# Suffix products instead of reciprocals in a linear attention with two dense layers, r made on VectorE, and a new order of the beginning

## The reference

```python
# r, k, v, w: (4, 8, 768, 48) float32, w in 0.8..0.95; u: (8, 48)
state = zeros(4, 8, 48, 48)
for t in range(768):
    cur = outer(u * k[t], v[t])
    y[t] = r[t] @ (state + cur)
    state = w[t][:, None] * state + outer(k[t], v[t])
x = y as (3072, 384)
h = x @ w_in                       # (384, 2048)
x = (h * clip(h + 3, 0, 6) / 6) @ w_out
xn = x / sqrt(mean(x * x) + 1e-6) * rms_g
out = (silu(xn @ w_gate) * (xn @ w_val)) @ w_out2   # 384 -> 1536 -> 384
```

## Time and profile before

| | |
|---|---|
| median of 3 runs | 933.13 us (932.55 to 935.83) |
| the profiled execution | 935.66 us, its span 933.9 us |
| TensorE matmuls busy | 921.6 us, 99% of the span |
| VectorE, ScalarE, GpSimd busy | 521.3, 361.7, 291.9 us |
| mean granted clock of TensorE | 0.998 of full |
| DMA | 60.4 MB, 65 GB/s over the span |

### The profile page before, as it was taken

How to read it: one execution, slowest core, us unless ns; L and a number is a source line. 1 busy time by engine, 2 the same in 40 slices (tenths; PEclk the granted TensorE clock), 3 DMA queues, 4 the chain that set the end, 5 groups by cost and what they waited for, 6 DMA issues and landing times.

```text
span 933.9 us, 17547 instructions
## 1 busy us (share of the span) xinstructions
PE 921.6 (99%) x7064; PEld 772.9 (83%) x7064; DVE 521.3 (56%) x752; ACT 361.7 (39%) x786; POOL 291.9 (31%) x244
## 2 busy tenths in 40 slices
PE   7999999999999999999999999999999999999998
PEld 7899988888888888888888888888888888888886
DVE  6888976566666666315774553553463373363332
ACT  4557454354444445336463123223223223223212
POOL 4789544454454444324351011011011001101000
PEclk9999999999999999999999999999999999999999
DMA  9874442233223231014221010010000001000000
GB/s 255 237 208 129 109 131 60 63 105 86 75 61 107 69 83 51 22 39 135 86 83 45 0 35 34 1 34 34 0 34 35 1 19 50 0 1 34 1 1 34
DMA packets 33008, 60.40 MB, mean 65 GB/s; under 512 B 6112, under 2 KB 19936, under 8 KB 32928
## 3 DMA queue, kind: packets, MB, share of 16 engines
q1 hardware_dynamic: 27104, 50.82, 18.7%
q10 hardware_dynamic: 5824, 8.47, 3.1%
HBM read 47.66 MB, written 9.44 MB: 61 GB/s over the span
## 4 chain that ended last, share of the span: by engine, by line
PE 93%; DVE 4%; issue 1%; DMA 1%; ACT 1%; SPq 1%; DVEq 0%; ACTq 0%
PE acc L1079 34%; PE bank L1050 11%; PE bank L1052 11%; PE bank L1051 11%; PE pair L1050 5%; PE pair L1051 5%; PE pair L1052 5%; DVE ki L731 1%; PE acc L1113 1%; PE pair L1132 1%; PE pair L1189 1%; PE pair L1161 1%; DVE cum L719 1%; PE bank L1068 1%; PE bank L1153 1%
## 5 line engine op out<-in xcount | busy, mean ns | idle before, releaser
L1079 PE MATMUL acc<-gs,w_dn 128*128 128x512 f32 (+1 forms) x1512 | 357.0, 382 | 1.2 <-issue 1.2
L1079 PEld LDWEIGHTS acc<-gs,w_dn 128*128 128x128 f32 x1512 | 272.9, 188 | 55.1 <-issue 1.3
L945 POOL TENSOR_TENSOR gs<-act_g,gs 128x512 fp32r<-128x512 f32 (+1 forms) x96 | 122.1, 1272 | 208.3 <-ACT gs L550 208.2
L1050 PE MATMUL bank<-xs,w_up 128*128 128x512 f32 (+1 forms) x459 | 171.9, 374 | 1.4 <-DVE state L762 1.2
L1052 PE MATMUL bank<-xs,w_up 128*128 128x512 f32 (+1 forms) x459 | 169.1, 368 | 0.0
L1051 PE MATMUL bank<-xs,w_up 128*128 128x512 f32 (+1 forms) x459 | 169.0, 368 | 0.0
L801 DVE SCALAR_TENSOR_TENSOR act_g<-act_u,bank 128x512 f32<-128x512 f32 (+1 forms) x112 | 67.5, 603 | 139.8 <-ACT act_u L542 139.8
L869 DVE TENSOR_TENSOR act_u<-act_u,bank 128x512 f32<-128x512 f32 x72 | 49.5, 688 | 146.8 <-ACT act_u L612 146.8
L542 ACT ACTIVATE act_u<-bank,half 128x512 f32<-128x512 f32 (+1 forms) x112 | 70.0, 625 | 150.8 <-PE bank L1052 139.9
L616 ACT ACTIVATE gs<-act_g 128x512 fp32r<-128x512 f32 x72 | 45.5, 632 | 155.9 <-DVE act_g L875 155.9
L1050 PEld LDWEIGHTS bank<-xs,w_up 128*128 128x128 f32 x459 | 86.4, 188 | 18.0 <-DVE state L762 1.6
(11 more groups left out here) (121 smaller groups left out, 1121.6 us busy)
## 6 DMA issues: line engine op xcount, KB each, us to landing
rkn<-in_rkN SPq DMA_DIRECT2D x22, 384.0 KB, 4.1
rkt<-in_rkT SPq DMA_DIRECT2D x44, 192.0 KB, 3.6
val<-in_valN SPq DMA_DIRECT2D x22, 256.0 KB, 3.0
x<-x_dram SPq DMA_DIRECT2D x6, 768.0 KB, 4.2
dec<-in_decT SPq DMA_DIRECT2D x46, 97.5 KB, 2.3
x_dram<-xo SPq DMA_DIRECT2D x5, 768.0 KB, 4.1
out<-xo SPq DMA_DIRECT2D x5, 768.0 KB, 3.3
raw_dn<-in_w_out SPq DMA_DIRECT2D x14, 192.0 KB, 4.8
```

The lines of the kernel that those rows point to most:

```text
L945: pool.tensor_tensor(gs[:, f % GRING, 1, tok], act_g[:, f % 2, tok], gs[:, f % GRING, 0, tok].bitcast(F32), ALU.subtract).then_inc(s_glo, 1)
L1050: pe.matmul(dst, w_hi, x_hi, start=first, stop=False)
L1079: last = pe.matmul(ps_o[m][:, tok], w[:, wp, m * P:(m + 1) * P], gs[:, f % GRING, xp, tok], start=f == 0 and a == 0, stop=f == nf - 1 and ...
```

## The change

For each group VectorE now scans the decay backwards (`prep_suffix`), which gives for each token the product of the decays after it (`after`) and for the whole chunk (`whole`). k is multiplied by the first. One small reciprocal of `whole` (8 columns) starts a second, forward scan (`prep_prefix`) whose result, cum / whole, is written over `dec` and multiplied with r. So four reciprocals of 128 columns leave, one scan comes in. r is made by VectorE (`prep_r` there, in phase PREP behind `prep_k`) for groups 2 and later; GpSimd makes it for groups 0 and 1. The state is scaled by the `whole` of the group that comes next, for all groups.

The order of the beginning changes. TensorE: the 30 unused products become 3 wide and 7 narrow ones; `sums(0)` goes behind the first hidden product, `keys(1)` into step 2. ScalarE: `place_val3`, the copy of the keys of group 0 and half of the fills of group 1 go to VectorE, the keys of group 1 to step 2. VectorE: `update_state(0)` and `scale_state(0)` go into steps 0 and 2. Loads: ScalarE issues w_in 0 to 2 and u and no more; SP issues the decay of group 2, waits for both masks (`s_mask` 2), and issues all else behind them. The decay is always loaded with 64 rows in the half 0 (130 KB instead of 97.5), and the decay of group g + 4, no longer g + 5, is loaded in INV1(g).

```diff
@@ sync
-                need(sp, s_cum, g - 1)
+                need(sp, s_rd, g - 1)
...
                 if phase == INV1:
-                    if g + 5 < GROUPS:
-                        load_dec(g + 5)
                     if g + 4 < GROUPS:
+                        load_dec(g + 4)
                         load_rk(g + 4)
...
             sp.dma_start(rms_s[:, :], rms_g).then_inc(ldG, 16)
-            landed(sp, ldR, 1, 2)
-            for b in range(PB):
-                sp.dma_start(u_b[T * b:T * (b + 1), :], u[b].partition_broadcast(T)).then_inc(ldU, 16)
+            load_dec(2)
+            sp.wait_ge(s_mask, 2)
             load_rkn(2)
-            load_dec(2)
+            load_up(sp, EARLY_UP)
+            load_dn(sp, 0)
             load_rk(2)
-            sp.wait_ge(s_ki, 2)
-            for f in range(FIRST_UP, FIRST_UP + 2):
+            load_dn(sp, 1)
+            for f in range(EARLY_UP + 1, FIRST_UP + 2):
                 load_up(sp, f)
                 load_dn(sp, f - 2)
             load_dec(3)
...
@@ scalar
-            for f in range(FIRST_UP):
+            for f in range(EARLY_UP):
                 load_up(act, f)
-                if f < 2:
-                    load_dn(act, f)
+            for b in range(PB):
+                act.dma_start(u_b[T * b:T * (b + 1), :], u[b].partition_broadcast(T)).then_inc(ldU, 16)
...
-            for g in range(2):
-                copy_bonus(g)
-                for part in range(2):
-                    fill_bonus(g, part)
-                place_val3(g)
-                if g == 0:
-                    copy_keys(0)
-            for g in range(2):
-                keep_last(g)
-            for f in range(2):
-                split_up(f)
+            copy_bonus(0)
+            for part in range(2):
+                fill_bonus(0, part)
+            copy_bonus(1)
+            fill_bonus(1, 0)
+            split_up(0)
             x1_hi(0, 0)
-            split_up(2)
+            split_up(1)
             x1_hi(1, 0)
-            copy_keys(1)
-            for f in range(3, FIRST_UP):
+            for f in range(2, FIRST_UP):
                 split_up(f)
...
@@ vector
+                backwards = (t.rearrange("p a b t -> p (a b t)")[:, ::-1] for t in (
+                    dec[0:DP, q, :, :, :], first1[0:DP, :, :, :]))
+                dve.tensor_tensor_scan(suffix[0:DP, q, 0:CHUNKS][:, ::-1], *backwards, 1.0,
+                                       ALU.mult, ALU.add).then_inc(s_suf, 1)
...
+            def prep_prefix(g):
+                q = slot(g)
+                dve.wait_ge(s_suf, g + 1)
+                need(dve, s_cum, g)
+                dve.reciprocal(whole1[0:DP, :, :, 0:1].rearrange("p a b t -> p (a b) t"), whole(g)).then_inc(s_inv, 1)
+                dve.wait_ge(s_inv, g + 1)
                 dve.tensor_tensor_scan(*(t.rearrange("p a b t -> p (a b t)") for t in (
-                    cum[0:DP, q, :, :, :], dec[0:DP, q, :, :, :], first1[0:DP, :, :, :])), 1.0,
+                    dec[0:DP, q, :, :, :], dec[0:DP, q, :, :, :], whole1[0:DP, :, :, :])), 1.0,
                                        ALU.mult, ALU.add).then_inc(s_cum, 1)
-                for p in ((0,), (1, 2, 3))[part]:
-                    dve.reciprocal(ki[0:DP, q, p, :, :], cum[0:DP, q, p, :, 1:T1]).then_inc(s_inv, 1)
...
+            def prep_r(g):
+                q = slot(g)
+                dve.wait_ge(s_cum, g + 1)
+                dve.wait_ge(p_y, g - 1)
+                dve.tensor_tensor(rd[0:DP, q, :, :, :].rearrange("p a b t -> p (a b) t"),
+                                  rkt[0:DP, q, 0, :, :, :].rearrange("p a b t -> p (a b) t"),
+                                  dec[0:DP, q, :, :, 0:T].rearrange("p a b t -> p (a b) t"), ALU.mult).then_inc(s_rd, 1)
...
                         prep_k(g + 2)
+                        prep_r(g + 2)
                 if phase == INV1 and g + 3 < GROUPS:
-                    prep_scan(g + 3)
-                if phase in (INV1, INV2) and g + 3 < GROUPS:
-                    prep_inv(g + 3, phase - INV1)
+                    prep_suffix(g + 3)
+                if phase == INV2 and g + 3 < GROUPS:
+                    prep_prefix(g + 3)
...
             for g in range(2):
-                mask_scores(g)
+                place_val3(g)
+            copy_first_keys()
+            mask_scores(0)
+            fill_half()
+            mask_scores(1)
             for g in range(2):
                 x1_lo(g, 0)
-            update_state(0)
             for f in range(NF1):
                 hidden(0, f)
                 if f == 0:
-                    prep_scan(2)
-                if f < 2:
-                    prep_inv(2, f)
+                    update_state(0)
+                    prep_suffix(2)
+                if f == 1:
+                    prep_prefix(2)
                 if f == 2:
+                    scale_state(0)
                     sum_bonus(2)
                     prep_k(2)
+                    prep_r(2)
...
@@ tensor
             pe.wait_ge(s_ones, 1)
-            busy(20)
+            busy(3, 4)
+            busy(5, 1)
             bonuses(0)
-            busy(3)
             pe.wait_ge(const, NCONST)
             scores(0)
             keys(0)
-            busy(3)
+            busy(2, 1)
             bonuses(1)
-            pe.wait_ge(s_bonus, 1)
-            sums(0)
-            busy(4)
             scores(1)
             outputs(0)
             outputs(1)
-            pe.wait_ge(s_bonus, PLACED)
-            keys(1)
```

More of the change, by code:

```diff
@@ L212, in columns, with after, whole @@
             return slice(g % B * C, (g % B + 1) * C)
-        def is_first(g):
-            return g < SETS
+        def after(g):
+            return suffix[0:DP, slot(g), 2:2 + CHUNKS].rearrange("p (c t) -> p c t", t=T1)[:, :, 0:T]
+        def whole(g):
+            return suffix[0:DP, slot(g), 0:CHUNKS].rearrange("p (c t) -> p c t", t=T1)[:, :, 1:2]
         def has_state(g):
@@ L513, in keep_last @@
             def keep_last(g):
-                act.wait_ge(s_cum, g + 1)
-                act.activation(last[0:DP, g % LASTS, :], cum[0:DP, slot(g), :, :, T:T1].rearrange("p a b t -> p (a b t)"),
-                               ACT.Copy).then_inc(s_last, 1)
+                act.wait_ge(s_suf, g + 1)
+                act.activation(last[0:DP, g % LASTS, :].unsqueeze(2), whole(g), ACT.Copy).then_inc(s_last, 1)
             def copy_keys(g):
@@ L736, in prep_k @@
                 landed(dve, ldR, g, 2)
-                dve.wait_ge(s_inv, PAIRS * (g + 1))
-                dve.tensor_tensor(*(t.rearrange("p a b t -> p (a b t)") for t in (
-                    ki[0:DP, q, :, :, :], rkt[0:DP, q, 1, :, :, :], ki[0:DP, q, :, :, :])), ALU.mult).then_inc(s_ki, 1)
+                dve.wait_ge(s_suf, g + 1)
+                need(dve, p_sc, g - 1)
+                keys_taken(dve, p_kt, g - 2)
+                dve.tensor_tensor(ki[0:DP, q, :, :, :].rearrange("p a b t -> p (a b) t"),
+                                  rkt[0:DP, q, 1, :, :, :].rearrange("p a b t -> p (a b) t"), after(g), ALU.mult).then_inc(s_ki, 1)
+            def prep_r(g):
[5 more added lines that the diff above has]
+                                  dec[0:DP, q, :, :, 0:T].rearrange("p a b t -> p (a b) t"), ALU.mult).then_inc(s_rd, 1)
             def mask_scores(g):
@@ L846, in attention @@
                 if phase == PREP:
-                    if has_state(g) and not is_first(g):
+                    if has_state(g):
                         scale_state(g)
@@ L884, in _ @@
             dve.memset(first1[:, :, :, 0:1], 1.0).then_inc(s_first1, 1)
+            dve.memset(suffix[:, :, CHUNKS:CHUNKS + 2], 1.0).then_inc(s_const, 1)
+            dve.memset(whole1[:, :, :, 1:T1], 0.0).then_inc(s_const, 1)
             dve.wait_ge(s_first1, 2)
             dve.tensor_scalar(ones[:, :].rearrange("p (b t) -> p b t", b=PB), first1[:, 0, :, 1:T1], 0.0, 1.0, ALU.mult, ALU.add).then_inc(s_ones, 1)
+            dve.wait_ge(s_const, 2)
             for g in range(2):
-                prep_scan(g)
-                for part in range(2):
-                    prep_inv(g, part)
+                prep_suffix(g)
+                prep_prefix(g)
                 prep_k(g)
@@ L966, in prep_r @@
                 pool.wait_ge(s_cum, g + 1)
-                need(pool, p_y, g - 1)
                 pool.tensor_tensor(*(t.rearrange("p a b t -> p (a b) t") for t in (
-                    rd[0:DP, q, :, :, :], rkt[0:DP, q, 0, :, :, :], cum[0:DP, q, :, :, 0:T])), ALU.mult).then_inc(s_rd, 1)
+                    rd[0:DP, q, :, :, :], rkt[0:DP, q, 0, :, :, :], dec[0:DP, q, :, :, 0:T])), ALU.mult).then_inc(s_rd, 1)
             def attention(phase, g):
@@ L1235, in run1 @@
                             keys(g + 1)
+                    if (e, f) == (0, 0):
+                        pe.wait_ge(s_bonus, PLACED)
+                        sums(0)
                     if (e, f) == (0, 2):
-                        sums_read(pe, 0)
+                        keys(1)
```

85 lines of the change are left out of this document (41 added, 44 removed).

## The result

The changed kernel takes 941.09 us (median of 6 runs, 939.46 to 941.54 without one disturbed run) against 933.3 us (median of 6) of the kernel before. The ratio is 1.007, 95% interval 1.0054 to 1.0085: slower by 5 to 8 us. The two medians differ by 7.8 us, but 85 later runs of the kernel before have medians of 934.5 to 934.7 us, so that the 6.5 us of the ratio is the better size. I had forecast 933.8 us and a range of 928.8 to 937.5; both the time and the likeliest case (no change that can be measured) were wrong.

The account below looks back on a forecast made before the run. TensorE, busy 921.6 of 933.9 us, was taken to bound the kernel. Terms of +2.0 (transfers), +0.5 (half clock), -1.2 (state waits) and -0.6 (instruction wait) gave +0.7 on 933.13: 933.8 us, range 928.8 to 937.5.

Parts of the forecast that it names:

- the likeliest case: Whole kernel: no measurable change, an effect below about 0.5% (4.7 us); chance 0.72, against faster 0.15 and slower 0.13.
- Masks: Beginning, VectorE in line with GpSimd: second mask ends at some 18.0 us against 17.7 before, bounds 17.0 and 20.2.
- First hidden product: Beginning, TensorE: starts at about 19.5 us instead of 22.66, if its wait for instructions is gone.
- the instruction wait: Beginning, TensorE stopped from 17.71 to 20.46 us, read as waiting for instructions behind data: 2.75 us, expected gone.
- Transfers: Loads behind SP's wait: piece 6 of w_in lands at 32.5 us, 5.5 later; step 5 starts +2.0 us, bounds -4.5 and +4.2.
- Clock: Half clock after TensorE idles 3 to 4 us ahead of group 1's sums: +0.5 us, bounds 0 and +1.7.
- The 0.5 us that I had for piece 7: Steps before step 5: piece 7 of w_in lands 2.3 us behind piece 6, delaying step 5 by 0.5 us more.
- 60 to 120 us: TensorE's waits there: VectorE's state waits go, -1.2 us (0 to -1.8); half an instruction wait goes, -0.6 (-1.2 to +1.2).
- 120 us on: Steady part to 560 us: VectorE's saving of 1.4 us per group is worth nothing, since TensorE is full.
- Sum: Whole kernel: +2.0 + 0.5 - 1.2 - 0.6 = +0.7 us on the median 933.13, giving 933.8 us.
- Rival B: SP's wait opens late, since VectorE loses to GpSimd and masks end at 20.2 us: +5.9, 939.0 us; chance 0.08.
- Rival A: Early start is kept, by transfers in time or masks by 17.0 us: 927.4 us, partly lost 930; chance 0.18.

Follow-up runs that it names:

- e12: The kernel before with only its unused TensorE products cut, from 30 of 128 columns to 3 of 512 and 7 of 128; 932.52 us, ratio 0.9974.
- e1: The changed kernel with SP waiting for its loads for r and k of group 1 instead of for both masks; 934.48 us, ratio 1.0009.
- e3: The kernel before with one line added: SP waits for both masks ahead of its loads for group 2; 936.53 us, ratio 1.0018.
- e11: The changed kernel, its wait for both masks kept, with 28 unused TensorE products of 256 columns instead of 3 of 512 and 7 of 128; 940.10 us.

## Why the prediction was wrong, point by point

**Masks.** Forecast 18.0 us, measured 18.15. Working through the line of VectorE and GpSimd was right within 0.6 us at every row. By the Trainium skill (SBUF — State Buffer, SBUF: two separate sides) such instructions lock each other out; the trace agrees, with 2.30 us for a scan of 1.23. I had missed one place: two copies of 96 columns, one input each, took 1.29 us beside GpSimd's r, where I had 0.5.

**First hidden product.** Forecast 19.5, measured 20.57 us; the instruction wait went as forecast. The outputs ran at 1.2 GHz, which I had not forecast.

**Transfers: the first of two terms that failed in size.** This is the term for piece 6 (32.5 us) in the +2.0 us. The place and the chain were right: piece 6, ScalarE's split, the fills, the 3.6 us gap ahead of the sums of group 1. I had +2.0 us for the start of step 5, without the clock; measured +4.5 with it. Piece 6 landed at 34.0 us instead of 32.5. The rate was no cause: the engines moved 271 GB/s from 18.2 to 34.0 us, where I had 262. That is 4.28 MB, and only 3.38 MB stood ahead of piece 6. I took the queue as served in order of issue. The landings are in that order (the next transfer, issued at 26.64 us, landed at 34.5), but by these bytes 0.9 MB of the transfers issued behind piece 6 must have been moved before it was whole: +3.3 us at this rate, worked out and not seen packet by packet. The mean of 271 GB/s holds the idle start already, so my 1.6 us for that and 0.4 us for the rate come off, which leaves 1.3 of the 1.5 us.

**Clock: the second.** I had +0.5 us, for six products. The half clock lasted from 35.5 to 42.2 us and covered three blocks: the sums of group 1 took 1.03 us instead of 0.61, the products of w_out behind them 2.37 instead of 1.64, and step 5's own products put its activation 1.0 us further back (5.5 us late, the first product 4.5). So the half clock behind the 3.6 us gap cost some 2.2 us, four times what I took and above my bound of 1.7. From the start of the fills to step 5 it took 4.2 us before and 5.74 here (34.45 to 40.19); 0.4 us of the difference are not the clock but the copy of the keys of group 1 in ScalarE's queue, a term that I had left out though the change puts it there. The 0.5 us that I had for piece 7 was not paid. This closes the step: 2.5 forecast, + 1.5 for the transfers, + 1.7 for the clock, + 0.4 for the copy, - 0.5, is 5.6, and 5.5 was measured.

**60 to 120 us.** Forecast -1.2 for the state and -0.6 for the instruction wait, measured -1.0 for both together. The wait for the state did not go (1.0 us in two waits), the instruction wait of 1.2 us did. e12 makes the same stretch from step 5 to pass 2 in 81.5 us with the old arithmetic, the changed kernel in 82.5, e1 in 81.8, before in 83.5. So the cheaper VectorE work, for which I had -1.2 us, gave nothing there that can be shown; the 1.2 us instruction wait explains what was gained. That this one went is luck in my sum, where it stood at half its size.

**120 us on.** No effect, as forecast, up to the last output copy: there the two traces are 4.5 us apart, and 4.4 at pass 2.

**Sum.** In the span: +5.5 at step 5, -1.0 to pass 2, and 0.8 at the very end. This last is in every version with the new arithmetic: the span ends 2.8 to 3.1 us after SP's last issue in these eleven, and 2.2 us in before, e3 and e12. In the same eleven, and not in the three, a packet of another instruction queue (q14) runs beside the last output. That it is the cause is not shown, but the 0.8 us go with the program's instructions and not with the beginning, and no term of mine had them. The two medians of six differ by 7.8 us and not by 5.3, since before's profiled execution was 2.4 us above its median. Rival B had 939.0 us, but its mechanism, late masks, did not occur. Rival A did not occur either; in e1, without the wait, the early start is kept, and the median is only that of before.

**Rivals of the explanation.** That the clock of the beginning was the cause is refuted by e11, where it stays up and the loss stays too, and by e1, where the loss goes with the clock still down for 6.7 us. That the wait for the masks protects the instruction fetch is refuted by e1 for the changed kernel; in the kernel before it does so (e3). Why is e1 3.6 us ahead of before at pass 2, and its median no better? Its profiled execution was its fastest (932.73 us, 1.75 below its median), before's lay 1.0 above that of the set, and 0.8 us are lost at the end: together 3.6 us. What the slower executions of e1 lose, and where, was not seen.

## What to carry to other kernels

A wait put ahead of prefetches is paid by the consumer with the least spare time (piece 6 had 0.5 us, and in the changed kernel the last 3.8 us of waiting cost 5.2), the more so where an in-order queue processes the prefetch ahead of urgent work; price the clock behind the new gap as well. When a change bundles a saving on engines that don't bound with a new order of the beginning, judge the two apart: the saving of 31 us on VectorE was worth nothing that could be shown, and taking one line out of the new order gave back all of the loss. The same line in the kernel before stretched the same steps by as much and cost only 2 us, since it also let TensorE's instructions through: read what a line does from the stretch in which it acts. In a beginning full of DMA, count TensorE's instructions too.

## What was not expected of the hardware

- TensorE's granted clock fell to 0.50 at 11.5 us, behind 3.5 us in which matmuls were busy 2.16 us, and stayed there until 25.1 us, while TensorE was 94% busy by the profile. By the Trainium skill (TensorE: Matmul & The Clock Gate, Part 1) half rate is the state after idling and full rate comes back with sustained work; here 12.67 busy us in 13.50 did not bring it back, where in e1 it came back at 19.6 us, behind 6.47 busy us in 6.70.
- Of the kernel before and e12 the one with the longer half clock (6.8 us against 3.4) is the faster: 932.52 against 934.48 us.
- A 192 KB transfer took 8.6 us from issue to landing with 271 GB/s moving, 2.8 us more than the same piece before.
- TensorE stood still for 2.75 us in the middle of a loop behind 441 recorded instructions, for 0.98 us behind 440 when 80 were taken out ahead of it, and not at all when the data queues were empty as its 16 KB instruction packet ran.
